# The product of the weights' remainder with the 64 rest channels, on 64 array rows

## The reference

```python
w = np.exp(weight_gen - np.max(weight_gen, axis=-1, keepdims=True))
w = w / (np.sum(w, axis=-1, keepdims=True) + 1e-09)
out = np.einsum('bshk,bskhg->bshg', w, x_unf)      # x_unf: windows of 7 tokens
x = out.reshape(B * S, D)
h = x @ w_in                                       # 192 -> 2048
g = h * (1.0 / (1.0 + np.exp(-1.702 * h)))
return (g @ w_out).astype(np.float32)              # 2048 -> 192
```

## Time and profile before

| | us |
|---|---|
| median of three runs | 1275.63 |
| span of the profiled execution | 1272.1 |
| its own time outside the span | not recorded; the median is 3.5 above the span |
| PE busy | 1209.2 (95%) |
| PE weight loads busy | 1095.6 (86%) |
| DVE busy | 841.0 (66%) |
| ACT busy | 621.3 (49%) |

### The profile page before, as it was taken

The page is one execution under the profiler, slowest core; times in us unless marked ns, Lnnn a source line. Parts: engine busy times, 40 slices in busy tenths (PEclk is TensorE's granted clock), DMA queues, the critical chain, the costliest instruction groups (busy, mean ns, idle before and its releaser), DMA issues.

```text
span 1272.1 us, 18060 instructions
## 1 busy us (share of the span) xinstructions
PE 1209.2 (95%) x6848; PEld 1095.6 (86%) x6848; DVE 841.0 (66%) x1066; ACT 621.3 (49%) x786; POOL 28.0 (2%) x14
## 2 busy tenths in 40 slices
PE   0398999999999999999999999999999999999998
PEld 0287899999999999999999999999999999999998
DVE  1997766666776666676666677666667666667732
ACT  0357644454454455454445445445545444544443
POOL 0321000000000000000000000000000000000000
PEclk9999999999999999999999999999999999999999
DMA  4400000000000000000000000000000000000000
GB/s 129 177 1 26 25 26 0 25 25 25 25 25 12 12 25 25 25 25 25 0 25 25 25 25 25 12 12 25 25 25 25 25 0 25 25 25 25 13 13 13
DMA packets 12590, 33.93 MB, mean 27 GB/s; under 512 B 1192, under 2 KB 3492, under 8 KB 12448
## 3 DMA queue, kind: packets, MB, share of 16 engines
q1 hardware_dynamic: 12576, 33.73, 8.0%
HBM read 21.14 MB, written 12.58 MB: 27 GB/s over the span
## 4 chain that ended last, share of the span: by engine, by line
PE 90%; DVE 6%; DMA 2%; ACT 1%; issue 0%; POOL 0%; SPq 0%; DVEq 0%; ACTq 0%; POOLq 0%
PE acc L494 30%; PE acc L496 14%; PE hid L474 9%; PE hid L478 9%; PE hid L476 9%; PE hid L475 9%; PE hid L479 9%; DMA xwin<-in_x 2%; DVE prod L320 2%; DVE sums L327 1%; PE hid L445 1%; DVE gate_lo L402 1%; DVE tap_max L349 1%; PE hid L448 1%; DVE conv_rest L335 0%
## 5 line engine op out<-in xcount | busy, mean ns | idle before, releaser
L494 PE MATMUL acc<-w,gate_hi 128*128 128x384 f32 x2048 | 603.7, 359 | 4.4 <-DVE outs L391 4.4
L402 DVE TENSOR_TENSOR gate_lo<-gate,gate_hi 128x1024 fp32r<-128x1024 f32 x256 | 314.5, 1228 | 373.0 <-ACT gate_hi L271 373.0
L268 ACT ACTIVATE gate<-hid 128x1024 f32<-128x1024 f32 x256 | 263.4, 1029 | 564.9 <-PE hid L479 564.8
L496 PE MATMUL acc<-w,gate_lo 128*128 128x192 f32 x2048 | 517.4, 253 | 0.0
L496 PEld LDWEIGHTS acc<-w,gate_lo 128*128 128x128 f32 x2048 | 391.4, 191 | 10.1
L494 PEld LDWEIGHTS acc<-w,gate_hi 128*128 128x128 f32 x2048 | 386.1, 189 | 15.7 <-DVE gate_lo L402 4.8
L271 ACT ACTIVATE gate_hi<-hid 128x1024 fp32r<-128x1024 f32 x256 | 261.5, 1021 | 0.0
L474 PE MATMUL hid<-xt_hi,w_hi 128*128 128x512 f32 x512 | 210.4, 411 | 3.1 <-DVE xtr L375 2.3
L478 PE MATMUL hid<-xtr,w1r_hi 128*128 128x512 f32 x512 | 203.8, 398 | 0.0
L475 PE MATMUL hid<-xt_lo,w_hi 128*128 128x512 f32 x512 | 201.9, 394 | 0.0
L476 PE MATMUL hid<-xt_hi,w_lo 128*128 128x512 f32 x512 | 201.7, 394 | 0.0
(11 more groups left out here) (32 smaller groups left out, 364.3 us busy)
## 6 DMA issues: line engine op xcount, KB each, us to landing
out<-outs SPq DMA_DIRECT2D x32, 384.0 KB, 2.4
xwin<-in_x SPq DMA_DIRECT2D x31, 384.0 KB
taps<-in_weight_gen SPq DMA_DIRECT2D x1, 3248.0 KB, 19.5
w_raw<-in_moe_w_out SPq DMA_DIRECT2D x1, 1536.0 KB, 13.5
w_raw<-in_moe_w_in SPq DMA_DIRECT2D x2, 512.0 KB, 7.8
w1r_raw<-in_moe_w_in SPq DMA_DIRECT2D x4, 256.0 KB, 12.5
xwin<-in_x SPq DMA_DIRECT2D x1, 768.0 KB
xwin<-in_x SPq DMA_DIRECT2D x4, 139.5 KB
```

What stands on the lines that cost most here:

```text
L268: nc.scalar.activation(gate[:, m % 2, :], hid[:, s, :, :], ACT.Gelu_apprx_sigmoid).then_inc(gate_ready, 1)
L402: nc.vector.tensor_tensor(gate_lo[:, i, :], gate[:, m % 2, :], gate_hi[:, i, :], ALU.subtract).then_inc(gate_lo_ready, 1)
L494: nc.tensor.matmul(acc[:, t, 0:2 * D], gate_hi[:, i, g], w2[:, c, :], start=(c == 0), stop=False)
L496: last = nc.tensor.matmul(acc[:, t, D:2 * D], gate_lo[:, i, g], w2[:, c, 0:D], start=False, stop=(c == CH - 1))
```

## The change

The product of the weights' remainder with the rest channels (L479 before) is done on 64 array rows instead of 128. Chunk 0 of the pair uses rows 0 to 63 of `w1r_lo` and of `xtr` (the `hi` of the rest channels); chunk 1 uses rows 64 to 127 of `w1r_lo` and of a new tensor `xtr_hi`, which holds the same `hi` in its lower half. The two stand one behind the other at the end of the pair's first product, and write to two banks. The product of `w1r_lo` with the `lo` of the rest channels is no longer computed.

ACT fills `xtr_hi` with two more instructions a tile; a new semaphore `rest_doubled` counts them, and DVE (ahead of its two subtractions into `xtr`) and PE wait for it. `conv` and `conv_rest` have one buffer in place of two, and the convolution's last addition waits for the transposes of the tile just ahead of its own instead of those one tile further back.

```diff
-        conv = sb("conv", [P, 2, TT, P])
-        conv_rest = sb("conv_rest", [P, 2, TT, REST])
+        conv = sb("conv", [P, TT, P])
+        conv_rest = sb("conv_rest", [P, TT, REST])
+        xtr_hi = sb("xtr_hi", [P, 2, NTOK], F32R)
...
+        rest_doubled = sem("rest_doubled")
...
                 for e in range(2):
                     nc.scalar.activation(rest_of(xtr, 0, b, e), rest_raw(s, e), ACT.Copy).then_inc(xt_hi_ready, 1)
+                for e in range(2):
+                    nc.scalar.activation(rest_of(xtr_hi, REST, b, e), rest_raw(s, e), ACT.Copy
+                                         ).then_inc(rest_doubled, 1)
...
-                        wait(dve, xt_raw, j - 1)
+                        wait(dve, xt_raw, j)
...
                 wait(dve, xt_hi_ready, 3 * j + 3)
+                wait(dve, rest_doubled, 2 * j + 2)
...
                 if m == 0:
                     wait(pe, xt_lo_ready, 3 * (j + 1))
+                    wait(pe, rest_doubled, 2 * (j + 1))
...
                         wait(pe, xt_lo_ready, 3 * (j + 2))
+                        wait(pe, rest_doubled, 2 * (j + 2))
...
                     nc.tensor.matmul(to, w1r_hi[:, f], xtr[:, b, :], start=False, stop=False)
-                    last = nc.tensor.matmul(to, w1r_lo[:, f], xtr[:, b, :], start=False, stop=True)
+                for e in range(2):
+                    rows = slice(e * REST, (e + 1) * REST)
+                    f = slice((2 * m + e) * P, (2 * m + e + 1) * P)
+                    last = nc.tensor.matmul(hid[:, s, e, :], w1r_lo[rows, f], (xtr_hi if e else xtr)[rows, b, :],
+                                            start=False, stop=True)
                 last.then_inc(hid_ready, 1)
```

More of the change, by code:

```diff
@@ L332, in conv_step @@
                         dve.wait_ge(conv_op, base + q)
-                        wait(dve, xt_raw, j - 1)
+                        wait(dve, xt_raw, j)
                     part = slice(P, D) if rest else slice(0, P)
-                    nc.vector.tensor_tensor((conv_rest if rest else conv)[:, b, :, :],
+                    nc.vector.tensor_tensor((conv_rest if rest else conv)[:],
                                             *(v.rearrange("p (t d) -> p t d", d=D)[:, :, part]
@@ L444, in transposes @@
                 for t in range(TT):
-                    nc.tensor.transpose(hid[:, s, 0, t * P:(t + 1) * P], conv[:, b, t, :], ident[:])
+                    nc.tensor.transpose(hid[:, s, 0, t * P:(t + 1) * P], conv[:, t, :], ident[:])
                 for t in range(0, TT, 2):
                     last = nc.tensor.transpose(hid[:, s, 1, t // 2 * P:(t // 2 + 1) * P],
-                                               conv_rest[:, b, t:t + 2, :].rearrange("p t d -> p (t d)"), ident[:])
+                                               conv_rest[:, t:t + 2, :].rearrange("p t d -> p (t d)"), ident[:])
                 last.then_inc(xt_raw, 1)
```

## The result

The changed kernel takes 1316.70 us (four runs, 1315.55 to 1317.42), the kernel before 1275.66 us beside it: a ratio of 1.0321, with a 95% interval of 1.0306 to 1.0335. The change makes the kernel 3.2% slower, 41.0 us. The spans differ by 1313.7 - 1272.1 = 41.6 us.

The account below looks back on a forecast made before the run. PE's stream was taken to bound the kernel. Changes of shape less overlap, +46 us, and +0.8 us in the first tile gave +47 us on 1275.6, so 1322.6 us, range 1219 to 1370 us.

Parts of the forecast that it names:

- PE's stream sets the time: PE, busy 1209.2 of 1272.1 us: a nanosecond between two of its matmuls counts in full, 256 times if once per pair.
- The halves work at the same time: The pair's two 64-row matmuls share one slot of 0.23 us, gaining 0.23 us a pair, 59 us by count of slots.
- The middle case: The second 64-row half starts a weight load (0.09 us) behind the first; gain 0.14 us a pair, 36 us.
- The change of shape: 128 to 64 rows and back each pair drains the array: 0.41 us, less 0.23 gained, +0.18 a pair, +46 us.
- the guess that one load of the two stays covered: Of a pair's two changes only one exposes its weight load: 0.16 + 0.25 = 0.41 us a pair.
- The signs named ahead: L469 to L473 and L473 to L489: 0.23 us no drain, 0.39 load ready, 0.48 load exposed; pair 4.80 us.
- only the matmul waits: At a change of shape on PE the weight load is already there: 0.39 - 0.23 = 0.16 us per change.
- load and matmul wait: Upper end at a change on PE: the load waits for the last matmul's recorded end; 0.25 us per change.
- The transposes' row: At a tile's border PE goes from matmul to transpose without cost; by that row alone the sum would be -59 us.
- The split, the copies, the buffer: ACT's copies, 0.77 us a tile, are covered except +0.8 us once in the first tile; one conv buffer costs 0.
- No drain: Rival: changes of shape on PE are free and the halves overlap; -36 to -59 us, 1217 to 1241 us; chance 34%.
- No overlap, with or without a drain: Two rivals, PE's halves run one after the other: no drain 1276.4 us, 6%; each change drains, 1358 to 1404 us, 6%.

Follow-up runs that it names:

- the runs on the number of changes: Against the changed kernel: each chunk's 64-row matmul behind its full-row ones, four changes a pair, 1473.16 us; two pairs' 64-row matmuls together, half the changes, 1276.82 us.
- the same order with 128 rows: Against the kernel before: remainder matmuls of two pairs together, on 128 rows, but tiles 0 and 1 in the old order; 1277.10 us, ratio 1.0019.
- A grouped order: Remainder matmuls of two pairs together in all tiles, on 128 rows: 1285.92 us, against 1276.37 us for the ungrouped run with 128 rows.

## Why the prediction was right, step by step

**PE's stream sets the time.** Right. PE's busy time grew by 41.5 us and the span by 41.6.

**The halves work at the same time.** Right, and shown three ways: equal starts in the rows, no change with one half left out, and 59.4 us more when both use the same half. The middle case, a second half trailing by 0.09 us, didn't occur. The Trainium skill (TensorE: Matmul & The Clock Gate, Part 3) puts the starts of matmuls on different row groups about 4 ns apart. The trace agrees: here the two rows read 0.00 to 0.01 us apart. Taken alone that rule would have forecast the wrong sign.

**The change of shape.** The mechanism was right as far as the rows reach: a matmul with another number of rows, and its load, wait, which takes away the overlap with the matmul ahead. That the array is empty by then isn't shown directly, since the ends are modelled; the load's constant 0.07 us ahead of the recorded end, behind 512 columns, behind 192 and at 1.2 GHz, speaks for it. A change costs 0.20 us in and 0.20 us out, 0.39 to 0.40 a pair. Predicted were 0.16 and 0.25, 0.41 in all. The sum was met, its parts were not: the guess that one load of the two stays covered was wrong. Both loads wait, but neither for the full recorded end of the matmul ahead: 0.33 us behind L469's start and not 0.39. The signs named ahead therefore read neither 0.39 nor 0.48 us, but 0.33 from L469 to L473 and 0.42 from L473 to L489, as these rows start with their loads; the pair, 4.78 us against 4.80 predicted, was the sign that held. So 0.20 lies between "only the matmul waits" (0.16) and "load and matmul wait" (0.25) on both sides, and that +46 came out near +41 is in part luck. Per pair it is 0.39 - 0.23 = 0.16, by the tiles' period 0.166, against the 0.18 of the sum; times 256 that is 42 us. With the 1.6 us of the other parts it would be 44, and 41.0 were measured (39.0 to 42.7 by the interval). In the first tiles PE's waits took up some of it: the one for DVE's `outs` fell from 4.4 to 3.9 us, the one for ACT's gate from 0.6 to 0.2. The rest of the difference stays open. The Trainium skill (TensorEngine Tiling (Array Packing), Key Properties) says that changing the tiling mode drains TensorE. The runs agree, at 0.20 us a change.

**The transposes' row.** That it says little about a change of rows was right. That it shows no cost was read too smoothly: from L474 to L475 it is 654.00 - 653.69 = 0.31 us there, against 0.25 behind a 192-column matmul elsewhere (606.28 to 606.53), and no other matmul of 128 columns is there to compare the transposes with.

**The split, the copies, the buffer.** Right in the steady part, not in tile 1. There is no new wait of PE from tile 2 on. DVE waited 0.79 us a tile for ACT's last copy (24.5 us in all) with 1.6 us of cover. In the first tile PE waited 3.14 us instead of 2.32, the 0.8 predicted. What I missed is the split done during tile 1: I read the cover from a tile in the steady part, while in tile 1 ACT is late and has none, which costs another 0.8 to 0.9 us. All these parts together cost 1.6 us.

**The rivals.** No drain (1217 to 1241 us) falls with the runs on the number of changes. No overlap, with or without a drain (1276 us, 1358 to 1404 us), falls with the same-half run, which is what no overlap would look like: 1376 us.

## What to carry to other kernels

Halves of the array used side by side are worth a whole slot (0.23 us for 512 columns at 2.4 GHz, in this kernel's fp32r), but each change between 128 and 64 rows costs nearly one (0.20 us). Count the changes, not the matmuls: one slot saved for two changes loses, two slots saved for two changes win a little (1269.8 against 1274.8 us, and against 1277.1 us for the same order with 128 rows). In a profile, look at the weight loads: where a load no longer starts with the previous matmul and waits for nothing named, its cover is gone.

## What the runs showed of the hardware that was not expected

A change costs the same 0.20 us going in and going out of the 64 rows, and the load behind it begins before the recorded end of the matmul ahead, 0.33 us after its start with an end recorded at 0.40. The lead is 0.07 us behind 192 columns too, and at 1.2 GHz, where the change costs 0.29 us. Behind a matmul of 192 columns the way in is 0.03 us cheaper; why stays open. With two waits of PE within 6 us, 2.52 and 3.27 us, the granted clock stood at its lower level for some 10 us in one run, and with nearly the same waits (2.47 and 3.68 us) for some 3 us in another. A grouped order that costs 0.03 us a tile in the steady part lost 9.6 us, most of it to PE's waits in the first two tiles.
